# Sums of squares for an RMS norm: blocks turned and added by VectorE, row groups joined by one short fp32 matmul, in place of six transposes

## What is computed

```python
# attention: batch 8, heads 8, seq 576, head_dim 64, 32 packed queries
p_packed = sm_attn(p, k, v)
out = sm_attn(q, p_packed, p_packed)          # q attends to the 32 packed rows
x = out.transpose(0, 2, 1, 3).reshape(4608, 512)
rms = np.sqrt(np.mean(x * x, axis=-1, keepdims=True) + 1e-06)
xn = x / rms * rms_g
g = xn @ w_gate                               # 512 x 1536
silu = g * (1.0 / (1.0 + np.exp(-g)))
x = silu * (xn @ w_val) @ w_out               # 1536 x 512
h = (x @ w1) * (x @ w2) @ w3                  # second block, 512 x 1024, 1024 x 1024
return h @ w_out2
```

## Time and profile before

| | us |
|---|---|
| median of 3 runs | 1325.72 (1324.65 to 1327.18) |
| the profiled execution's own time | 1326.28 |
| its span, first to last instruction | 1324.7 |
| PE busy | 1313.4 |
| DVE busy | 874.1 |
| ACT busy | 410.9 |
| POOL busy | 121.6 |

### The profile page before, as it was taken

The page is one execution under the profiler, slowest core; times in us unless marked ns, Lnnn a source line. Parts: engine busy times, 40 slices in busy tenths (PEclk is TensorE's granted clock), DMA queues, the critical chain, the costliest instruction groups (busy, mean ns, idle before and its releaser), DMA issues.

```text
span 1324.7 us, 21669 instructions
## 1 busy us (share of the span) xinstructions
PE 1313.4 (99%) x8590; PEld 1090.2 (82%) x8590; DVE 874.1 (66%) x1371; ACT 410.9 (31%) x785; POOL 121.6 (9%) x92
## 2 busy tenths in 40 slices
PE   9999999999999999999999999999999999999998
PEld 7778878888878788887888899788888888888886
DVE  4768666576575765756754667866766686677665
ACT  5344533434434334343333433211200120112000
POOL 0100101001000010010100531100200010020000
PEclk9999999999999999999999999999999999999999
DMA  9673435353534434333326486745454345545202
GB/s 355 233 276 124 157 122 166 126 160 109 169 98 164 159 117 162 124 119 104 115 74 233 164 313 260 279 142 183 128 175 159 128 128 190 175 145 192 92 1 64
DMA packets 117202, 211.40 MB, mean 160 GB/s; under 512 B 33904, under 2 KB 35952, under 8 KB 114032
## 3 DMA queue, kind: packets, MB, share of 16 engines
q1 hardware_dynamic: 90672, 203.21, 44.4%
q10 hardware_dynamic: 26432, 6.82, 2.2%
HBM read 168.04 MB, written 41.96 MB: 159 GB/s over the span
## 4 chain that ended last, share of the span: by engine, by line
PE 95%; DMA 1%; DVE 1%; issue 1%; ACT 1%; POOL 0%; SPq 0%; DVEq 0%; ACTq 0%; POOLq 0%
PE psum L965 8%; PE psum L967 8%; PE psum L966 8%; PE psum L853 8%; PE psum L855 7%; PE psum L854 7%; PE psum L879 7%; PE psum L878 7%; PE psum L877 7%; PE psum L1007 4%; PE psum L1009 4%; PE psum L1008 4%; PE psum L798 3%; PE psum L819 1%; PE psum L782 1%; PE psum L824 1%
## 5 line engine op out<-in xcount | busy, mean ns | idle before, releaser
L853 PE MATMUL psum<-a_hi,m_hi 128*128 128x288 f32 x768 | 235.5, 307 | 1.4 <-DVE g_s L1553 0.8
L854 PE MATMUL psum<-a_lo,m_hi 128*128 128x288 f32 x768 | 226.3, 295 | 0.0
L855 PE MATMUL psum<-a_hi,m_lo 128*128 128x288 f32 x768 | 226.3, 295 | 0.0
L853 PEld LDWEIGHTS psum<-a_hi,m_hi 128*128 128x128 f32 x768 | 144.2, 188 | 47.4 <-issue 39.8
L1553 DVE SCALAR_TENSOR_TENSOR g_s<-g_s,psum 128x288 f32<-128x288 f32 x192 | 86.6, 451 | 129.1 <-ACT g_s L1261 128.9
L879 PE MATMUL psum<-g_hx,wo_lo 128*128 128x512 f32 x384 | 152.0, 396 | 0.0
L878 PE MATMUL psum<-g_hx,wo_hi 128*128 128x512 f32 x384 | 151.4, 394 | 0.0
L1268 ACT CAST g_hx<-g_h 128x288 fp32r<-128x288 f32 x192 | 83.1, 433 | 219.7 <-DVE g_h L1559 214.4
L877 PE MATMUL psum<-g_hx,wo_hi 128*128 128x512 f32 x384 | 150.5, 392 | 0.1
L854 PEld LDWEIGHTS psum<-a_lo,m_hi 128*128 128x128 f32 x768 | 144.3, 188 | 5.2
L855 PEld LDWEIGHTS psum<-a_hi,m_lo 128*128 128x128 f32 x768 | 144.1, 188 | 0.0
(11 more groups left out here) (187 smaller groups left out, 2413.5 us busy)
## 6 DMA issues: line engine op xcount, KB each, us to landing
w_in<-in_w_gate SPq DMA_DIRECT2D x24, 1024.0 KB, 7.3
w_in<-in_w_val SPq DMA_DIRECT2D x24, 1024.0 KB, 5.1
wb_hi<-w_scratch SPq DMA_DIRECT2D x56, 256.0 KB, 2.8
wb_lo<-w_scratch SPq DMA_DIRECT2D x56, 256.0 KB, 3.0
w_hi<-w_scratch SPq DMA_DIRECT2D x49, 256.0 KB, 2.8
w_lo<-w_scratch SPq DMA_DIRECT2D x49, 256.0 KB, 3.7
kT<-in_kT SPq DMA_DIRECT2D x8, 1152.0 KB, 7.3
v_sb<-in_v SPq DMA_DIRECT2D x8, 1152.0 KB, 10.0
```

What stands on the lines that cost most here:

```text
L853: nc.tensor.matmul(in_ps[which], hi, a2_hi[:, t, par, :], start=par == 0, stop=False)
L854: nc.tensor.matmul(in_ps[which], hi, a2_lo[:, t, par, :], start=False, stop=False)
L855: last = nc.tensor.matmul(in_ps[which], lo, a2_hi[:, t, par, :], start=False, stop=par == 1)
```

## The change

- `fold(a, t)` on VectorE, new: when GpSimd has written half t of wsum, `transpose` turns each 32 x 32 block of its 128 x 288 numbers into wz[:, 0], and `tensor_reduce` adds each turned row of 32 into 128 x 9 numbers, kept in the first 9 columns of that half of wsum. They are sums over 32 of the 128 rows; four partitions hold the four parts of a token.
- SS on TensorE: one fp32 matmul with weights sel (128 x 32: four identities of 32 on top of each other) and 18 moving columns, output 32 x 18, in place of six transposes. It waits for both folds of the batch (part_ready).
- SS on VectorE: scale and epsilon work on 32 x 18 numbers, without the reduction; GpSimd's power works on 32 x 18 in place.
- The tokens stand in r_dram in another order (token 32 b + i at 18 i + b), so `scale_a2` reads r_sb with a stride of 18.
- fold of half 0 stands in slot 17 and that of half 1 in slot 18 of VectorE, each right behind g_h and ahead of the low part of g_hx. In the prologue fold(0, 0) stands behind wf_evict(0) and fold(0, 1) behind fuse_split(1, 4).
- The product of the next Z waits for the fold of the half before (part_ready in place of wsum_ready).
- sel is made by VectorE at the start, from ident, ahead of the memset of mask.

```diff
-TP = 96
+TP = 32
+FOLD = (17, 18)
@@ GpSimd
             def inverse_rms(a):
                 pool.wait_ge(neg_ready, 1)
                 pool.wait_ge(ms_ready, a + 1)
-                if a:
-                    pool.wait_ge(r_stored, 16 * a)
-                nc.gpsimd.tensor_tensor(rr[:], ms[:], neg_half[:], ALU.pow).then_inc(rr_ready, 1)
+                nc.gpsimd.tensor_tensor(rr[:], rr[:], neg_half[:].to_broadcast([TP, NT]), ALU.pow).then_inc(rr_ready, 1)
...
-                nc.gpsimd.tensor_tensor(a2T[:, t, :, :], a2T[:, t, :, :],
-                                        r_sb[:, HALF * t:HALF * (t + 1)].unsqueeze(1).to_broadcast([P, 2, HALF]),
+                blocks = HALF // TP
+                scale = r_sb[:].rearrange("p (i b) -> p b i", b=NT)[:, blocks * t:blocks * (t + 1), :]
+                half = a2T[:, t, :, :].rearrange("p a (b i) -> p a b i", i=TP)
+                nc.gpsimd.tensor_tensor(half, half, scale.unsqueeze(1).to_broadcast([P, 2, blocks, TP]),
                                         ALU.mult).then_inc(a2s_ready, 1)
@@ TensorE
                 if kind == "SS":
-                    pe.wait_ge(wsum_ready, 2 * (a + 1))
-                    for j in range(NT):
-                        last = nc.tensor.transpose(xy[j // 3][0:TP, j % 3 * P:(j % 3 + 1) * P],
-                                                   wsum[:].rearrange("p (i j) -> p j i", j=NT)[:, j, :], ident[:])
+                    pe.wait_ge(part_ready, 2 * (a + 1))
+                    pe.wait_ge(sel_ready, 1)
+                    last = nc.tensor.matmul(xy[0][0:TP, 0:NT], sel[:], parts_ss, start=True, stop=True)
@@ VectorE
                 if kind == "SS":
                     full(dve, "SS", a, part)
                     if a:
-                        dve.wait_ge(msum_ready, a)
-                    nc.vector.tensor_reduce(ssum[:].rearrange("p (a j) -> p a j", a=2),
-                                            psum[0:TP, 6:8, 0:3 * P].rearrange("p a (j n) -> p a j n", n=P), AX.X, ALU.add).then_inc(xy_free, 1)
+                        dve.wait_ge(r_stored, 16 * a)
+                    nc.vector.tensor_scalar(rr[:], psum[0:TP, bank, 0:NT], 1.0 / DM, 0.0, ALU.mult, ALU.max).then_inc(xy_free, 1)
                     freed(dve, "SS", a, 0)
...
+            def fold(a, t):
+                dve.wait_ge(wsum_ready, 2 * a + t + 1)
+                turned = wz[:, 0, :]
+                nc.vector.transpose(turned, wsum[:, HALF * t:HALF * (t + 1)]).then_inc(turned_ready, 1)
+                dve.wait_ge(turned_ready, 2 * a + t + 1)
+                nc.vector.tensor_reduce(parts_ss[:, t, :], turned.rearrange("p (b n) -> p b n", n=TP), AX.X, ALU.add).then_inc(part_ready, 1)
...
+            dve.wait_ge(const_ready, 2)
+            nc.vector.tensor_reduce(sel[:], ident[:].rearrange("p (g n) -> p n g", n=TP), AX.X, ALU.add).then_inc(sel_ready, 1)
             nc.vector.memset(mask[:], 0.0).then_inc(mask_clear, 1)
...
             wf_evict(0)
+            fold(0, 0)
             fuse_split(1, 3)
             item("Z", 0, 1)
             fuse_split(1, 4)
+            fold(0, 1)
             item("SS", 0, 0)
...
+                if b + 1 < B and s in FOLD:
+                    fold(b + 1, FOLD.index(s))
                 if b + 1 < B and s in NORM2:
```

More of the change, by code:

```diff
@@ L150, in build @@
         ones = const("ones", [P, 1])
-        neg_half = const("neg_half", [TP, NT])
+        neg_half = const("neg_half", [TP, 1])
         gcol = const("gcol", [P, HC])
@@ L155, in build @@
         rden1 = const("rden1", [P, 2])
-        ssum = const("ssum", [TP, NT])
+        sel = const("sel", [P, TP])
         GROUPS2 = 2 * HALF // NP
@@ L159, in build @@
         den2, rden2 = const("den2", [P, GROUPS2]), const("rden2", [P, GROUPS2])
-        ms, rr = const("ms", [TP, NT]), const("rr", [TP, NT])
+        rr = const("rr", [TP, NT])
         with ExitStack() as st:
@@ L312, in build @@
         fuse_bank = [2, 3, 4, 5, 0, 1, 2, 3]
-        const_ready, neg_ready = sem("const_ready"), sem("neg_ready")
+        const_ready, neg_ready, sel_ready = sem("const_ready"), sem("neg_ready"), sem("sel_ready")
+        turned_ready = sem("turned_ready")
         mask_clear, mask_ready = sem("mask_clear"), sem("mask_ready")
@@ L328, in build @@
         gram_ready, s1_half, s2_half = sem("gram_ready"), sem("s1_half"), sem("s2_half")
-        ppg_ready, ssum_ready, msum_ready = sem("ppg_ready"), sem("ssum_ready"), sem("msum_ready")
+        ppg_ready, part_ready = sem("ppg_ready"), sem("part_ready")
         max2_ready, d2_ready, e2_ready, sum2_ready = sem("max2_ready"), sem("d2_ready"), sem("e2_ready"), sem("sum2_ready")
@@ L359, in build @@
         bres_act, bres_dve, out_stored = sem("bres_act"), sem("bres_dve"), sem("out_stored")
+        parts_ss = wsum[:].rearrange("p (t n) -> p t n", t=2)[:, :, 0:HALF // TP]
         number = item_numbers()
@@ L1348, in item @@
                     if 2 * a + part:
-                        dve.wait_ge(wsum_ready, 2 * a + part)
+                        dve.wait_ge(part_ready, 2 * a + part)
                     nc.vector.tensor_tensor(wz[:], psum[:, 6:8, 0:HALF], a2T[:, part, :, :], ALU.mult).then_inc(xy_free, 1)
@@ L1353, in item @@
                     if a:
-                        dve.wait_ge(msum_ready, a)
-                    nc.vector.tensor_reduce(ssum[:].rearrange("p (a j) -> p a j", a=2),
-                                            psum[0:TP, 6:8, 0:3 * P].rearrange("p a (j n) -> p a j n", n=P), AX.X, ALU.add).then_inc(xy_free, 1)
+                        dve.wait_ge(r_stored, 16 * a)
+                    nc.vector.tensor_scalar(rr[:], psum[0:TP, bank, 0:NT], 1.0 / DM, 0.0, ALU.mult, ALU.max).then_inc(xy_free, 1)
                     freed(dve, "SS", a, 0)
[L1358 to L1362, removed]
+                    nc.vector.tensor_scalar(rr[:], rr[:], EPS_RMS, None, ALU.add).then_inc(ms_ready, 1)
                 if kind == "M":
```

## The result

The changed kernel takes 1328.38 us (median of 20 runs, 1327.21 to 1331.53) against 1325.62 for the kernel before (20 runs, 1323.87 to 1327.88). The ratio is 1.0021, 95% interval 1.0015 to 1.0027. The forecast was 1326.1, with 1323.4 to 1329.2 as range: the time lies in the range, but 2.4 us of the 2.8 were not in the sum.

What follows compares the result with a forecast made beforehand. TensorE, busy 99% of the span, was taken as the bound. Steady batches -0.4, batch 0 +0.35 and the prologue +0.47 summed to +0.4 us, giving a median of 1326.1 us, range 1323.4 to 1329.2.

Steps and rivals of the forecast that it cites:

- TensorE is the bound: TensorE, busy 99% of the span, bounds the kernel everywhere; item SS's six transposes add 0.66 us to its chain.
- The new matmul: In item SS on TensorE: 0.10 on the way in, 0.22 itself, 0.20 on the way out, 0.52 us without a wait.
- Steady batches: Batches 1 to 6, slot 18: second fold 0.27 us behind TensorE's arrival, a gain of 0.07 each, -0.4 for six.
- Batch 0: First loop batch: VectorE is later there, the second fold ends 0.69 us behind TensorE's arrival, costing +0.35 us.
- The prologue: Before the loop: item SS waits for fold(0, 1), and M starts later by 0.47 us, bounds +0.2 and +0.7.
- What I cost at nothing: Behind the mean: a power of 1.3 to 4.0 us and strided scaling up to twice 1.48, among others, cost nothing.
- rival 2: Slot 17: the first fold pushes the product and everything behind it in every batch; sum +3.1 us, 1328.8; chance 0.13.
- Rival 3: Power to a_hi: power and scaling so slow that the cast comes late, up to 10 us in all, 1336; chance 0.03.
- Rival 1: Steady batches: folds come in time, no drain for 128 x 32; sum -2.1 to -2.8 us, about 1323.3; chance 0.16.
- The chances: For the whole time: faster 0.12, same (change under 0.2%, 2.65 us) 0.74, slower 0.14.

Runs made afterwards that it cites:

- e1: The changed kernel without the fold of half 1, item SS waiting only for the first fold and GpSimd's sum: 1326.39 us, ratio 1.0003 to the kernel before.
- e9: As e8, and in the prologue VectorE does fold(0, 1) ahead of fuse_split(1, 4): 1333.23 us, ratio 1.0050 to the kernel before.
- e10: The changed kernel with scale_a2 on the first 32 tokens of each half alone: 1327.00 us, ratio 1.0009 to the kernel before.
- e11: The kernel before with scale_a2 on the first 32 tokens of each half alone: 1326.58 us, ratio 1.0003 to the unedited kernel before.
- e7: The kernel before with one more power (96 x 12 numbers) on GpSimd ahead of its own: 1330.77 us, ratio 1.0032 to the kernel before.
- e8: The changed kernel with item SS in slot 19 of the loop in place of slot 18: 1333.21 us, ratio 1.0056 to the kernel before.

## Where the prediction was right, and what its sum lacked

- **TensorE is the bound, six transposes hold 0.66 us**: right.
- **The new matmul**: it is of the form 128*32 and waits at its load as assumed (0.62 us of idle load ahead of it, most of it the wait for the fold). I took 0.52 for it without a wait; e1 has 0.36. Sized too high, with no effect on the sum, as the wait covers the way in.
- **Steady batches, -0.07 each**: measured -0.045. **Batch 0, +0.35**: measured +0.35. The end of the second fold behind TensorE's arrival was forecast as 0.27 and 0.69, and measured as 0.28 and 0.68.
- **The prologue, +0.47**: measured +0.67. GpSimd's sum took the full 1.18 us, not my 1.0, because VectorE's fuse_split ran beside it (e9). TensorE also waited 0.33 us for wf_second, behind the late scaling, which I had put under cover of the last fuses.
- **"What I cost at nothing"**: here the prediction failed. The power lay within my bounds (3.21, between 1.3 and 4.0), the strided scaling too (1.82, under twice 1.48), and ScalarE's cast in the loop did not wait, as I said. But I only asked who waits for the scaling's result, not what runs beside it. Its new place, 228.0 in batch 1, meets VectorE's subtraction in slot 21 for almost its full length. The 1.02 us of that subtraction in the trace of before, against 0.46 in slot 17, showed the effect, and I did not read that row; "durations of VectorE repeat to 0.02 us here", said against rival 2, is wrong for it. Nor do 5.3 us for the way through DRAM hold, which takes 4.67 to 7.52. Put at nothing, this term is 1.5 to 2 us (e10, e11 and the traces).
- **Rival 2**, slower by 3.1 us, came out near in size by chance, not by its cause: slot 17 pushed nothing. **Rival 3** had the right start (power and scaling) and the wrong end. **Rival 1** is refuted: the fold came 0.28 late.
- The chances, 0.74 for within 0.2%, leant on a cover that I had not checked. The ratio of 1.0021 lies on the edge. The waits and their sizes were right by their mechanism; that the time still lies in the range is luck, since more than half of the loss was in no term of the sum and in no rival.

Not settled: from where on a held subtraction costs TensorE time. In the traces the loss goes with which instruction the scaling meets and for how long, and the landing of r_sb moves by up to 3 us between batches; I did not move it in steps. Nor is it settled whether the slow stores of rest_scratch have to do with the change.

## What to carry to other kernels

When an edit moves an instruction on GpSimd, list the VectorE instructions with two SBUF operands at its new place, and put them down as longer by up to its whole length: an engine off the critical path can lengthen one that is on it. A step that is put out of one engine's work in favour of a denser layout ([32, 18] for [96, 6]) must be priced at each later user of that layout. And a matmul that waits for a chain through two other engines pays back its saving where that chain is late by as much: here each steady batch saved 0.30 us without the wait (e1) and 0.045 with a second fold that was 0.28 late. Before a trace is set against another, look for waits in the one of before that are its own, such as the store above.

## What the runs showed of the hardware

- A subtraction on VectorE with both operands in SBUF, 0.45 us alone, took 1.75 when it began 0.28 us behind a scaling of GpSimd of 1.7 us. In the nine traces with full scalings on GpSimd 65 of these subtractions are longer than 0.52 us, and each of the 65 ends 0.31 to 0.33 us behind the end of a scaling. g_s and g_h, with an operand in PSUM, and the maximum of one operand were not lengthened. It goes both ways: GpSimd's sum of 0.81 took 1.18 beside VectorE's fuse_split. The Trainium skill ("SBUF — State Buffer", section "SBUF: two separate sides") says that the two share a port pair as an exclusive lock, and that a VectorE operation with two SBUF inputs takes part in it, against a GpSimd operation that reads SBUF; the traces agree with that.
- GpSimd's power goes by the columns of a partition and not by the numbers: 96 x 6 in 1.37 us, 32 x 6 in 1.36, 96 x 12 in 2.31 (e7), 32 x 18 in 3.25.
- A stride of 18 elements in one of two fp32 operands: VectorE 1.23 us for 576 columns in place of 0.75, GpSimd 1.82 in place of 1.50 on average.
- An fp32 matmul of 128 x 32 weights and 18 columns, with the change of form on both sides, costs TensorE 0.36 us between matmuls of 128 x 128 (e1), and 0.24 at its place in e8, between the gate matmuls and `outof`.
